# Hardware loops, a rounded copy moved from POOL to ACT, and another order of the attention work beside an MLP

## The reference

```python
mag = sqrt(a_re**2 + a_im**2); scale = minimum(mag, 0.999) / (mag + 1e-6)
a_re, a_im = a_re * scale, a_im * scale
for t in range(S):                       # S = 768; per batch (4) and head (8), D = 48
    new_re = ar * S_re - ai * S_im
    new_im = ar * S_im + ai * S_re       # ar, ai: step t of a_re, a_im, per row of the state
    S_re, S_im = new_re + outer(k[t], v[t]), new_im
    y[t] = q[t] @ S_re
x = y as (3072 tokens, 384)
x = relu(x @ w_in)**2 @ w_out            # d_ff 2048  (MLP1)
g = x @ w_gate; out = (silu(g) * (x @ w_val)) @ w_out2    # d_ff 1536  (MLP2)
```

## Time and profile before

| | |
|---|---|
| median of three runs | 1262.54 us |
| profiled execution | 1262.62 us, span 1260.8 us |
| mean granted TensorE clock | 0.978 |
| TensorE busy | 1191.2 us (94%) |
| DVE busy | 709.0 us (56%) |
| ACT busy | 690.8 us (55%) |
| POOL busy | 237.1 us (19%) |
| instructions fetched, queue q8 | 90 packets, 1.47 MB |

### The profile page before, as it was taken

How to read it: one execution, slowest core, us unless ns; L and a number is a source line. 1 busy time by engine, 2 the same in 40 slices (tenths; PEclk the granted TensorE clock), 3 DMA queues, 4 the chain that set the end, 5 groups by cost and what they waited for, 6 DMA issues and landing times.

```text
span 1260.8 us, 27340 instructions
## 1 busy us (share of the span) xinstructions
PE 1191.2 (94%) x11158; PEld 1125.8 (89%) x11158; DVE 709.0 (56%) x1154; ACT 690.8 (55%) x1345; POOL 237.1 (19%) x267
## 2 busy tenths in 40 slices
PE   2777999999999999999999989999999999999998
PEld 1665898998989989989989979999999999999998
DVE  4889778778787787788787601352232322222222
ACT  5777778778778777777777434532222222222221
POOL 1000333333323333323333424100000000000000
PEclk9966999999999999999999989999999999999999
DMA  4322111112211121112121032310010101010000
GB/s 143 117 94 70 39 40 58 58 51 59 70 53 63 39 58 58 40 58 58 50 59 46 8 113 73 124 37 19 20 35 4 38 1 38 1 38 20 1 19 20
DMA packets 42156, 62.76 MB, mean 50 GB/s; under 512 B 3120, under 2 KB 37680, under 8 KB 41648
## 3 DMA queue, kind: packets, MB, share of 16 engines
q1 hardware_dynamic: 42032, 61.01, 15.5%
HBM read 46.84 MB, written 14.16 MB: 48 GB/s over the span
## 4 chain that ended last, share of the span: by engine, by line
PE 69%; DVE 12%; ACT 12%; issue 5%; DVEq 0%; ACTq 0%
PE bank L1347 8%; PE bank L1348 8%; PE bank L1349 8%; PE bank L1366 4%; PE bank L1370 4%; PE bank L1368 4%; PE bank L1264 4%; PE bank L1266 4%; PE bank L1265 4%; PE bank L1277 3%; PE bank L1281 3%; PE bank L1279 3%; PE bank L1200 3%; PE bank L1190 2%; ACT L500 2%
## 5 line engine op out<-in xcount | busy, mean ns | idle before, releaser
L1083 DVE TENSOR_TENSOR prod<-bank,silu 128x384 f32<-128x384 f32 x96 | 53.5, 557 | 285.2 <-PE bank L1349 269.2
L751 ACT ACTIVATE silu<-bank 128x384 f32<-128x384 f32 x84 | 41.4, 493 | 280.9 <-PE bank L1349 280.9
L458 POOL CAST ghi<-rg 128x384 fp32r<-128x384 f32 x128 | 88.9, 695 | 547.7 <-ACT rg L634 547.7
L460 POOL TENSOR_TENSOR glo<-rg,ghi 128x384 fp32r<-128x384 f32 x128 | 144.8, 1131 | 10.3
L1264 PE MATMUL bank<-xhi,win_hi 128*128 128x384 f32 x384 | 134.8, 351 | 6.7 <-DVE xlo L988 3.8
L1277 PE MATMUL bank<-ghi,wout_hi 128*128 128x384 f32 x384 | 132.1, 344 | 0.0
L1266 PE MATMUL bank<-xhi,win_lo 128*128 128x384 f32 x384 | 130.3, 339 | 0.0
L1265 PE MATMUL bank<-xlo,win_hi 128*128 128x384 f32 x384 | 130.1, 339 | 0.0
L1281 PE MATMUL bank<-ghi,wout_lo 128*128 128x384 f32 x384 | 128.7, 335 | 0.0
L1279 PE MATMUL bank<-glo,wout_hi 128*128 128x384 f32 x384 | 128.5, 335 | 0.0
L631 ACT ACTIVATE rg<-bank 128x384 f32<-128x384 f32 x128 | 62.2, 486 | 69.8 <-PE bank L1266 68.9
(11 more groups left out here) (161 smaller groups left out, 2999.6 us busy)
## 6 DMA issues: line engine op xcount, KB each, us to landing
gates_sb<-in_gates SPq DMA_DIRECT2D x48, 192.0 KB, 2.5
qk_sb<-in_qk SPq DMA_DIRECT2D x24, 384.0 KB, 3.1
v_sb<-in_v SPq DMA_DIRECT2D x24, 192.0 KB, 3.2
xT_scratch<-yT SPq DMA_DIRECT2D x48, 96.0 KB, 2.5
xin<-xT_scratch SPq DMA_DIRECT2D x8, 576.0 KB, 4.1
y1T_scratch<-y1s SPq DMA_DIRECT2D x8, 576.0 KB, 3.5
x<-y1T_scratch SPq DMA_DIRECT2D x8, 576.0 KB, 4.0
out<-o_sb SPq DMA_DIRECT2D x8, 576.0 KB, 3.0
```

What stands on the lines that cost most here:

```text
L460: pool.tensor_tensor(glo[:, j % GR, :], rg[:, j % 2, :], ghi[:, j % GR, :].bitcast(F32), ALU.subtract)\
```

## The change

Three things are changed at once.

1. **Loops.** The Python loops over the steady units become hardware loops (`Fori`) on every engine: units 2 to 6 on TensorE, DVE, ACT and POOL (five rounds), two rounds of two units on SP, three rounds of two units in MLP2 on TensorE, DVE and ACT, and four rounds of a store and a load on SP. The values waited for are then computed in registers.
2. **ghi.** The rounded copy of rg moves from POOL (`high_low`) to ACT (`relu2`), as its third instruction; POOL keeps the subtraction (`low`).
3. **Order.** Within a chunk ACT, DVE and TensorE do the same work in another order.

```diff
 @@ sync @@
-            for b in range(1, B - 1):
+            with sp.Fori(1, B - 1) as b:
-            for u in range(1, NU - 3):
+            with sp.Fori(1, NU - 3) as u:
 @@ gpsimd @@
-            def high_low(base, j):
-                pool.wait_ge(mlp1["g"], base + j + 1)
-                pool.wait_ge(mlp1["out"], max(base + j + 1 - GR, 0))
-                pool.tensor_copy(ghi[:, j % GR, :], rg[:, j % 2, :]).then_inc(mlp1["hi"], 1)
+            def low(base, j):
                 pool.wait_ge(mlp1["hi"], base + j + 1)
                 pool.tensor_tensor(glo[:, j % GR, :], rg[:, j % 2, :], ghi[:, j % GR, :].bitcast(F32), ALU.subtract)
-            for u in range(2, NU - 1):
+            with pool.Fori(2, NU - 1) as u:
 @@ scalar, relu2 @@
                 act.activation(rg[:, j % 2, :], rg[:, j % 2, :], ACT.Square).then_inc(mlp1["g"], 1)
+                act.wait_ge(mlp1["g"], base + j + 1)
+                act.wait_ge(mlp1["out"], floor0(base + j + 1 - GR))
+                act.activation(ghi[:, j % GR, :], rg[:, j % 2, :], ACT.Copy).then_inc(mlp1["hi"], 1)
 @@ scalar, unit: order of a chunk (S0 is works(ci, (0,)), n + 1 but where given) @@
-    high_gates, S0, inverse, split_x, S1, signs, S2, weight1[0], S3, decays, S4, block_decays, angle,
-    S5, high_theta, S6, S7, copy32(n), copy64(n), weight1[1], weight1[2], squares(n+2), sines,
-    S8, evac_y(n), magnitudes(n+2), evac_Q, S9, evac_K, S10, evac_D
+    S0, high_gates, S1, inverse, weight1[0], signs, split_x, decays, S2, S3, block_decays, angle,
+    S4, high_theta, S5, copy32(n), S6, copy64(n), weight1[1], squares(n+2), S7, sines, weight1[2],
+    S8, evac_y(n), magnitudes(n+2), evac_Q, S9, evac_K, evac_D, S10
 @@ vector, unit @@
-    capped, clear_state, denominator, log_gates, to_borders8(n), to_borders16(n), low_gates,
-    to_borders32(n), split_x, weight1[0], in_block(n), ratio, to_borders64_Q(n), ...,
-    k_end, weight1[1], weight1[2], msq(n+2), decay_state(n), rotate, state(n), low_carry, rotate_end
+    capped, clear_state, log_gates, denominator, low_gates, to_borders8(n), ratio, to_borders16(n),
+    weight1[0], split_x, to_borders32(n), in_block(n), to_borders64_Q(n), ...,
+    k_end, weight1[1], msq(n+2), decay_state(n), rotate, state(n), rotate_end, weight1[2], low_carry
 @@ tensor, unit @@
-    S0 to S3, scores_mid(n), scores8(n), scores16(n), gate_sums, S4, block_sums, S5, S6, S7,
-    scores32(n), scores64(n), phase_sums, S8, outputs(n), S9, S10, state(n), transposes_Q, transposes_K
+    S0 to S3, gate_sums, scores_mid(n), scores8(n), scores16(n), block_sums, S4, S5,
+    scores32(n), scores64(n), S6, phase_sums, S7, S8, outputs(n), state(n), S9, S10,
+    transposes_Q, transposes_K
 @@ scalar, vector and tensor: steady units of MLP1, and of MLP2 @@
-            for u in range(2, NU - 1):
+            with act.Fori(2, NU - 1) as u:          # and dve.Fori, pe.Fori
-            for i in range(1, NU // 2 - 1):
+            with act.Fori(1, NU // 2 - 1) as i:     # and dve.Fori, pe.Fori
```

More of the change, by code:

```diff
@@ L467, in works @@
                         if kind == "up":
-                            high_low(unit_no * NF1, j)
+                            low(unit_no * NF1, j)
             def unit(u, has_tail=True, has_head=True):
@@ L480, in _ @@
                 if kind == "up":
-                    high_low((NU - 2) * NF1, j)
+                    low((NU - 2) * NF1, j)
             for j in range(NF1):
-                high_low((NU - 1) * NF1, j)
+                low((NU - 1) * NF1, j)
         @block.scalar
@@ L693, in unit @@
                         weight1(i)
+                    if has_next or ci < CPU - 2:
+                        squares(n + 2)
+                    works(ci, (7,), *flags)
+                    if nxt:
+                        sines(n + 1)
                     for i in pieces[2:3]:
                         weight1(i)
[L696 to L699, removed]
                     works(ci, (8,), *flags)
@@ L1030, in unit @@
                         weight1(i)
-                    for i in pieces[2:3]:
-                        weight1(i)
                     if has_next or ci < CPU - 2:
@@ L1039, in unit @@
                     if nxt:
+                        rotate_end(n + 1)
+                    for i in pieces[2:3]:
+                        weight1(i)
+                    if nxt:
                         low_carry(n + 1)
-                        rotate_end(n + 1)
             dve.wait_ge(s_const, 48)
@@ L1065, in _ @@
             unit(1, False)
-            for u in range(2, NU - 1):
+            with dve.Fori(2, NU - 1) as u:
                 unit(u)
@@ L1120, in _ @@
             unit2(1, 1)
-            for i in range(1, NU // 2 - 1):
+            with dve.Fori(1, NU // 2 - 1) as i:
                 unit2(i * 2, 0)
@@ L1302, in unit @@
                     works(ci, (0, 1, 2, 3), *flags)
+                    if nxt:
+                        gate_sums(n + 1)
                     scores_mid(n)
@@ L1306, in unit @@
                     if nxt:
-                        gate_sums(n + 1)
-                    works(ci, (4,), *flags)
-                    if nxt:
                         block_sums(n + 1)
-                    works(ci, (5, 6, 7), *flags)
+                    works(ci, (4, 5), *flags)
                     scores32(n)
                     scores64(n)
+                    works(ci, (6,), *flags)
                     if nxt:
                         phase_sums(n + 1)
-                    works(ci, (8,), *flags)
+                    works(ci, (7, 8), *flags)
                     outputs(n, ci, u)
+                    state(n, ci)
                     works(ci, (9, 10), *flags)
-                    state(n, ci)
                     if nxt:
@@ L1333, in _ @@
             unit(1, False)
-            for u in range(2, NU - 1):
+            with pe.Fori(2, NU - 1) as u:
                 unit(u)
@@ L1410, in _ @@
             unit2(1, 1)
-            for i in range(1, NU // 2 - 1):
+            with pe.Fori(1, NU // 2 - 1) as i:
                 unit2(i * 2, 0)
```

39 lines of the change are left out of this document (18 added, 21 removed).

## The result

The changed kernel takes 1314.36 us (median of four runs, 1312.84 to 1319.12) where before took 1262.42 beside it: slower, ratio 1.042 with a 95% interval from 1.039 to 1.045. The forecast had the sign and the direction of each part, but 14 us where 51.9 were measured; its range ended at 1297. The profiled execution took 1313.47 us, 1311.7 of it span, at a mean granted clock of 0.966.

What follows compares the result with a forecast made beforehand. The prediction took TensorE to set the pace in steady units and MLP2, and a DVE, ACT and TensorE chain in unit 0. 1262.6 + 9 (steady units) + 3 (unit 0) + 2 (loops) = 1276.6 us; range 1259 to 1297.

Steps and rivals of the forecast that it cites:

- MLP2 and the drain: After the attention units: nothing but MLP2's loops is edited, 0; the drain's added ACT copies raise ACT to 45 us busy.
- the term for the loops: Jumps back between rounds: 0.5 us each in MLP1's part, +2 us in all, mostly covered by 24 transposes; 0 in MLP2.
- upper bound of 3.6 us: Per jump, one code fetch in the open: 1.1 us a page plus 2.5 us for a small DMA; 22 for six.
- open jumps: Rival: each of six TensorE jumps costs 3.6 us in the open, ACT late behind it; 1296 us, chance 0.12.
- MLP2's loops at 0: MLP2's jumps cost nothing: ACT and DVE mostly idle, TensorE has 27 matmuls (4.7 us) behind a round's last wait.
- that stretch, new order, from the end of scores64: Steady chunk up to the Q copy: ACT's list takes 11.56 us, first half of Q usable 13.0 us behind scores64.
- The stalls that it gave for the Q copy: TensorE's K transposes in a steady unit wait 1.1 us in the third chunk, 0.8 in the first, none in the second.
- 77.8: ACT's busy time per steady unit with the added copy, up from 69.3 us by 8.5 us.
- 0.4 us: First chunk of a steady unit: DVE's borders come this much late for scores64 and phase_sums, +0.4 us.
- DVE should lose less: Without the casts POOL works 1.15 instead of 1.89 us per tile, easing DVE's contention; counted inside the lower bound.
- 1.4 to 1.5: Added us per steady unit from the Q copy's stalls and late borders; +9 us for six units.
- +3 for unit 0: Unit 0 and the first chunk after it: chunk 1 -0.6, chunks 2 and 3 +1.8 each; between -4 and +6 us.

Runs made afterwards that it cites:

- mid_loop: Kernel before, TensorE's units 2 to 6 a hardware loop, scores of 8 and 16 rows, middle scores and state cut to one head: 1230.8 us, single run.
- tiny_loop: Kernel before, TensorE's units 2 to 6 a hardware loop, scores of 8 to 64 rows, middle scores and state cut to one head: 1240.19 us.
- short_loop: Kernel before, TensorE's units 2 to 6 a hardware loop, scores of 8 and 16 rows and middle ones cut to one head: 1261.02 us.
- small_glo: Changed kernel, all loops written out, POOL's subtraction for glo in units 2 to 6 over 32 of 384 columns: 1271.03 us.
- old_first: Changed kernel, all loops written out, unit 0 alone in the order of before on ACT, DVE and TensorE: 1283.69 us.
- loops_only: Kernel before with hardware loops on SP, ACT, DVE and TensorE, POOL written out, no copy moved, no order changed: 1285.71 us.

## Why the prediction was right or wrong

**Right: which engine.** TensorE's stalls and gaps are the time; MLP2 and the drain did not move, as priced.

**Wrong, the largest: the term for the loops.** It had "0.5 us each, +2" for the four jumps of MLP1, since 24 transposes stand in front of a jump. They cover 0.7 us of a branch of 5.1 to 5.6 us: the first matmul of the next round comes 4.7 to 5.2 us after the transposes. The upper bound of 3.6 us, a page and the landing of a DMA that it called small (the row is of 192 KB), was too low too, and it had no term for the clock. Measured: 6.3 us a jump in the old order (gap 4.2, clock 1.9) and 7.4 in the new one. In the new order the gaps are 4.67 to 5.18 instead of about 4.2, and the stall before the scores of 64 rows in the chunk behind a jump is 0.94 instead of 0.37. In sum 30.8 us instead of 2, of which 25.8 to 27.6 are TensorE's MLP1 loop. The rival *open jumps* had the mechanism, and the rule of the Trainium skill, Runtime: NRT & Kernel Launch, section Instruction fetch mechanics, that a taken branch out of the resident pages must fetch first, is borne out for MLP1: 11 pages a round and a gap with a page fetched in it at each of four jumps. It is not for MLP2, mid_loop and tiny_loop, whose rounds are several pages long and jump back with none fetched. The 108 ns of the Trainium skill, Advanced Engine Details and Errata, section Control Flow Timing, were no price of such a jump; a taken one without a fetch took 207 to 243 ns on TensorE. But the rival, with 1296 us, charged all jumps alike, and six of them, where the loops have five: MLP2's has one.

**Right for too weak a reason: MLP2's loops at 0.** The prediction gave 27 queued matmuls as the cover. The runs show another cause: the body stays resident, and no page is fetched for it. mid_loop has that without any cover but the one that failed in short_loop. The prediction could have counted a round's matmuls and weight loads: the earlier trace rows give 1063 + 1062 for MLP1 and 2530 + 2528 for some eight units of MLP2, about 1270 in all for the two of a round. That would not have given the limit, but it would have told the two loops apart.

**Wrong in what it looked at: the steady unit.** The step "that stretch, new order, from the end of scores64" was worked out well: its list of ACT work came to 11.56 us, and on ACT's time line after it is 11.55, from 383.43 to 394.98, again without a gap:

```profile
383.43 0.47 ACT L628 ACTIVATE rg<-bank 128x384 f32<-128x384 f32 x1
...
384.92 0.76 ACT L594 ACTIVATE AT<-bank 32x256 f32<-32x256 f32 x2
...
394.98 1.05 ACT L569 ACTIVATE QT<-bank 96x512 f32<-96x512 f32 x2
```

The stalls that it gave for the Q copy, 1.1, 0.8 and 0 in the three kinds of chunk, are 0.75, 0.48 and 0. ACT is busy 77.3 us a unit; 77.8 was said. What failed is that the stretch ahead of scores64 was left out but for 0.4 us. There TensorE now has `gate_sums` and two slots less to do, while DVE's chain QA, KA, masks, KB, which TensorE waits for, is as long as ever: 6.0 us from the start of QA to the end of KB in both (356.91 to 362.92 before, 376.14 to 382.10 now). And the sentence that without the casts "DVE should lose less" was right for the sum and took the contention as an average. It is a matter of which instructions meet. Before, POOL had nothing from 357.5 to 364.1 in the third chunk, while DVE was busy 6.04 of 6.60 us with that chain; now glo falls on KA.

```profile
357.50:364.10 6.60, 6.53 (x43) 6.15 (x40) 6.04 (x11) 4.76 (x8) 0.00 (x0) 1.00 0.22 62
```

small_glo measured POOL's contention at 2.4 us a unit in this order, next to the 2.6 that the steady unit lost without loops, where 1.4 to 1.5 was forecast for other reasons.

**Unit 0 and the units at the ends.** The prediction had +3 for unit 0. By the table it is +1.3 to +1.5, and the traces of the experiments bear the sign out: in eleven executions unit 0 has the order of before and ends at 110.5 to 112.7 us, in six it has the new one and ends at 113.0 to 113.8. Its steps show: scores from 36.83 instead of 33.90, block_sums at 42.09 instead of 41.75, theta's product at 45.82 instead of 45.54, and the Q transposes 1.9 sooner, their wait 2.67 instead of 4.61:

```profile
36.83 1.98 PE L1189 MATMUL bank<-QT,KT 96*64 96x64 f32 x32
42.09 0.62 PE L1132 MATMUL bank<-t_r,sums_r 128*88 128x384 f32 x1
...
57.41 1.91 PE L1162 MATMUL bank<-ident,Qn 128*96 128x128 f32 x8 [2.67 <-DVE Qn L874]
```

Unit 1, which the sum did not count apart, lost 3.3 (up to 5 in other executions, see old_first), and the rest 1.5. Unit 7 has MLP1's works beside attention as well, so the sum should have had seven units and not six.

**Sum, as measured.** Steady order and copy, units 2 to 6: 13.2; unit 0: 1.3; unit 1: 3.3; the rest: 1.5; loops: four rounds at 7.44 more, 29.8; unit 2 of the looped kernel: 1.8. That is 50.9, the whole difference of span. The 1.8 stay open: in unit 2 one stall before the scores of 64 rows is 2.08 us, there with the other engines looping and not without, and no experiment took it apart. The extra 0.6 us of gap in the new order lies in the branches themselves, 5.08 to 5.58 us against 4.33 to 4.99 in loops_only; why they are longer there is open.

## What to carry to other kernels

Before a long unrolled body is made a loop, count the instructions of one round on the engine that sets the pace, weight loads included: here a round that did not stay resident paid a jump of some 5 us and then the clock, each time. And look at the branches in the trace, which give the price of a jump at once. When a helper engine's work moves in time, look at which instructions it will now run beside, not at its busy time: on another engine's critical product it can cost that product's own length again, as it did here. And work out both sides of a moved instruction, the stretch that ends with it as well as the one that begins there.

## What the runs showed of the hardware

- TensorE's loop: a round of 685 matmuls and 686 weight loads ran without a gap and with no instruction page fetched, its jump taking 208 to 243 ns; one of 811 + 811 stopped 4.0 to 4.4 us at every jump. The limit lies between, for bodies like these. The Trainium skill, Runtime: NRT & Kernel Launch, section Instruction fetch mechanics, gives TensorE room for 2048 instructions; the 811 + 811 recorded are under that and were refetched, so for this case the measured bound is the one to use. Nor were the two resident pages of which the prediction told the limit here: before, the 2125 matmuls and loads of a unit came in eight or nine pages, so by estimate mid_loop's 1371 fill more than five.
- The gap brings the clock down: twelve matmuls 0.32 us apart instead of 0.17 behind each, mean granted clock 0.55 in that window, and 1.00 in the next.
- A DVE product of 96 x 512 from two tiles took 675 to 681 ns alone and 1495 beside a POOL subtraction of 128 x 384; with 32 columns of the latter it took 736. In the row above, POOL's subtraction ran from 376.52 to 377.71 and the product from 376.75 to 378.25: 0.54 us beyond POOL's end, little less than its whole length alone. The Trainium skill, SBUF — State Buffer, section "SBUF: two separate sides", calls it an exclusive lock: a DVE operation with two SBUF inputs and a GpSimd operation that reads SBUF can't run together, and whichever starts second is blocked. The trace fits that to 0.14 us. The prediction had the contention in the earlier trace rows and did not ask where it would fall in the new order.
- The jumps of ACT and DVE, with bodies of 139 and 115 recorded instructions a unit in loops_only, cost nothing that could be seen in the old order (1285.7 against 1285.4 us); in the changed kernel their branches took 40 to 67 ns.
